# The seam between neighbouring pairs of an RWKV-style recurrence: first right sides around the low scores, turned answers and first answers ahead of the diagonal and the u-r scores

## The chip, the cores and the metric

The kernel runs on one core of one Trainium2 chip. The metric is the device time of one execution in microseconds (us). The core has TensorE (PE, with its weight loads PEld), VectorE (DVE), ScalarE (ACT), GpSimd (POOL) and SyncE (SP, which issues all the DMAs here). Each works through its own list in order, and they wait for each other by semaphores.

## What is computed

```python
def _attn_ref(r, k, v, w, a, b):           # 4 x 8 heads, 768 steps, head size 40
    for t in range(S):
        y[:, :, t] = np.einsum('bhd,bhde->bhe', rt, state)
        Sa = np.einsum('bhde,bhe->bhd', state, at)
        state_decay = state * wt[:, :, None, :] - np.einsum('bhd,bhe->bhde', Sa, bt)
        state = state_decay + np.einsum('bhd,bhe->bhde', vt, kt)
    return y
# x: y as (3072 tokens, 320)
# first MLP:  h = x @ w_in (2048);  x = (h - tanh(h)) @ w_out
# experts:    out = sum over 4 of  p_e * (relu(x @ w1[e]) @ w2[e]), inner size 1024
```

## The kernel before, in words

The sequence is cut into 6 chunks of 128 steps. A unit is one chunk of 4 heads; there are 48 units, worked in 24 pairs (pair `p` holds units `2p` and `2p+1`, called `j` = 0 and 1). Four pairs (`PPC`) make a chunk. Within a chunk the recurrence becomes a triangular system, solved in four blocks of 32 steps, b = 0 to 3. For each block and each `j` this chain runs:

- PE, `right_sides` (L569 with the state, L572 with the values) and, for b > 0, `right_side_rest` (L585, with the answers found so far and the low scores): the right side in a bank.
- DVE, `save_right_side` (L1052): right side to `rhs`.
- PE, `answer` (L595): `rhs` times the inverse of the diagonal block.
- ACT, `save_answer` (L868): answer to `un`.

Around that chain, per pair: `scores` (L708, L712) masked by DVE `mask_scores` (L1076); `scores_low` (L723), saved by ACT in three pieces (`save_low`, L885); `natural` (L736), saved by L892; `turn_state` (L610), saved by L874; `turn_answers` (L622), saved by ACT to `ut` (`save_turned_answers`, L879); `scores_ur` (L687, from `ut` and r), masked by DVE `mask_ur` (L1067); `state_by_values` (L634) and `state_by_answers` (L642), added by DVE `update_state` (L1061) and decayed by POOL (L1189); results (L658, L667, L675), saved by DVE (L1086).

`diagonal(i)` (L549) forms the diagonal blocks of a unit that was prepared some pairs ahead: DVE scan (L991) and reciprocal (L997), POOL scaling (L1178, L1181), diagonal on PE, `save_diagonal` on ACT (L863). Pairs 0 and 1 prepare three units each, pair 2 none, pairs 3 to 18 two each, later ones none; the diagonals follow one pair later.

The order on each engine is written out by hand. `program` calls, for p = 0 to 23, the engine's `pair(p)` and, at a chunk's end, its `mlp` for the chunk before. So pairs 7, 11, 15, 19 and 23 are followed by an MLP of 16 steps on PE (`drained(p)` is true for them), in which the u-r scores and results of that pair are finished (L814 up, L823 down). The other 19 seams p to p+1 join two pairs directly. On ACT a pair may end with more work: in pairs 3 to 6 `weight_hi`, the casts of two pieces of MLP weights (L900 to L902, which wait for DMAs), and in pairs 9, 13, 17 and 21 `tokens_hi`, the casts of turned tokens (L909, L910). After pair 3 DVE computes the rest of the inverses of the next chunk (L1027, L1030).

After the last MLP come the experts (L1383, L1393, ACT L1418, DVE L1448 and L1455), from about 830 us to the end.

At a direct seam PE's list before reads `scores_low(p+1)`, `turn_answers(p)`, both first right sides, a wait for `update_state`, one diagonal, `scores_ur(p)`, both first answers, both right sides of block 1, `turn_state`, the second diagonal, `right_side_rest` of block 1.

Of the kernel before, what the change touches and what calls it, by code (L numbers as in the profile page):

```python
# [142 lines left out]
def recurrence_and_first_mlp(nc, sem, pairs, ident, kbaw, rvt, vn, w_in, w_out, scratch, turned, middle):  # L143
    ctx = ExitStack()
    with ctx:
# [58 lines left out]
        def rows(s):  # L204
            return slice(HALF * s, HALF * s + HD)
# [5 lines left out]
        def block_of(b):  # L211
            return slice(BLK * b, BLK * (b + 1))
# [13 lines left out]
        def drained(p):  # L226

            return p % PPC == PPC - 1 and p >= PPC
# [306 lines left out]
        def _(pe):  # L535
            def diagonal(i):

                _, b_made, a_made, _ = parts(i)
                o = diagonal_of(i)
                pe.wait_ge(scaled, 2 * (i + 1))  # L540
                if i in late_diagonals:
                    pe.wait_ge(ut_saved, (i - FIRST) // 2 + 1)
                elif i >= FIRST:
                    pe.wait_ge(lt_saved, i)
                elif i >= 2:
                    pe.wait_ge(lt_saved, i - 1)
                for b in range(NB):
                    for h, q, s in heads:
                        mm = pe.matmul(o[block_of(h), block_of(b)], b_made[rows(s), 1, q, block_of(b)],  # L549
                                       a_made[rows(s), q, block_of(b)], start=True, stop=True)  # L550
                mm.then_inc(lt_full, 1)
# [198 lines left out]
            def pair(p):  # L750
                after_mlp = p > 0 and drained(p - 1)
                prepared = [] if after_mlp else prepared_in(p - 1)
                more = p + 1 < NP
                right_sides(p, 0, 0)
                right_sides(p, 1, 0)
                if after_mlp:
                    pe.wait_ge(x2_saved_v, 2 * (p // PPC - 1))
                    pe.wait_ge(x2_saved_a, 2 * (p // PPC - 1))
                if p:
                    pe.wait_ge(st_read, p)  # L760
                for i in prepared[:1]:
                    diagonal(i)
                if p and not after_mlp:
                    scores_ur(p - 1)
                answer(p, 0, 0)
                answer(p, 1, 0)
                right_sides(p, 0, 1)
                right_sides(p, 1, 1)
                turn_state(p)
                for i in prepared[1:2]:  # L770
                    diagonal(i)
                right_side_rest(p, 0, 1)
                right_side_rest(p, 1, 1)
                for i in prepared[2:]:
                    diagonal(i)
                state_by_values(p)
                answer(p, 0, 1)
                answer(p, 1, 1)
                if p and not after_mlp:
                    result_by_answers(p - 1)  # L780
                right_sides(p, 0, 2)
                right_sides(p, 1, 2)
                right_side_rest(p, 0, 2)
                right_side_rest(p, 1, 2)
                if more:
                    scores(p + 1, 0)
                answer(p, 0, 2)
                answer(p, 1, 2)
                result_by_keys(p)
                right_sides(p, 0, 3)  # L790
                right_sides(p, 1, 3)
                right_side_rest(p, 0, 3)
                right_side_rest(p, 1, 3)
                result_by_state(p)
                answer(p, 0, 3)
                answer(p, 1, 3)
                if more:
                    natural(p + 1, 0)
                    scores(p + 1, 1)
                state_by_answers(p)  # L800
                if more:
                    natural(p + 1, 1)
                    scores_low(p + 1)
                turn_answers(p)

            passes = [(HI0, HI0), (HI0, LO0), (LO0, HI0), (HI1, HI1), (HI1, LO1), (LO1, HI1), (ST2, ST2), (ST2, LO2)]

# [49 lines left out]
        def _(act):  # L857
# [62 lines left out]

            def pair(p):
                prepared = [] if p and drained(p - 1) else prepared_in(p - 1)
                for i in prepared[:1]:
                    save_diagonal(i)
                save_answer(p, 0, 0)
                save_answer(p, 1, 0)
                save_turned_state(p)
                for i in prepared[1:]:
                    save_diagonal(i)
                for b in range(1, NB):  # L930
                    save_answer(p, 0, b)
                    save_answer(p, 1, b)
                if p + 1 < NP:
                    save_natural(p + 1, 0)
                    save_natural(p + 1, 1)
                if p + 1 < NP:
                    save_low(p + 1)
                save_turned_answers(p)
                if 0 <= p - PIECES_FROM < PIECES // 2:
                    weight_hi(2 * (p - PIECES_FROM))  # L940
                    weight_hi(2 * (p - PIECES_FROM) + 1)
                if tokens_turned_in(p) is not None:
                    tokens_hi(tokens_turned_in(p))
# [555 lines left out]
```

## Time and profile before

| | |
|---|---|
| three timed runs | 1687.89 us median (1684.33, 1687.89, 1695.4) |
| the profiled execution | 1691.96 us, its span 1690.3 us |
| PE busy | 1485.6 us (88%) |
| PEld busy | 1295.8 us (77%) |
| DVE busy | 810.7 us (48%) |
| ACT busy | 421.0 us (25%) |
| POOL busy | 375.2 us (22%) |
| mean granted TensorE clock | 0.946 |

The span is the time from the first to the last instruction. Matmuls are pipelined, so a busy PE is not one at its peak. In the timeline a row is a run of like instructions: its start, how long it lasts, engine, line, operands, how many (matmuls of 32-bit numbers are shown as two), and in square brackets how long the engine had been idle before it and what released it. "Granted clock" is the share of 2.4 GHz that TensorE was allowed; it has two levels, 2.4 and 1.2 GHz.

### The profile page before, as it was taken

Reading aid. Unit: us, or ns where it says so; the run is one execution under the profiler, and the core shown is the slowest. Engines: PE = TensorE matmul, PEld = TensorE weight load, DVE = VectorE, ACT = ScalarE, POOL = GpSimd, SP = SyncE. Lnnn points to the kernel's source line nnn. Section 1 sums busy time; section 2 is a strip of 40 time slices with the busy share of each in tenths; the row PEclk is TensorE's granted clock in tenths of the full one; section 3 lists DMA queues with packets and bytes.
Section 4 is the critical chain, followed back from the end, with each engine's and each line's share of the span. In section 5 each row is a group of like instructions: output and inputs, shape, how many; then the busy total and the mean of one; then the engine's idle time right before and its main releaser. Section 6 shows DMA issues by size and latency. Waiting matters only on the chain. (4 is left out here: it accounts for less than half of the span.)

```text
span 1690.3 us, 37880 instructions
## 1 busy us (share of the span) xinstructions
PE 1485.6 (88%) x15888; PEld 1295.8 (77%) x15888; DVE 810.7 (48%) x1395; ACT 421.0 (25%) x859; POOL 375.2 (22%) x314
## 2 busy tenths in 40 slices
PE   1288466998998998999997789999999999999998
PEld 0166355876877886887786669999999999999998
DVE  6876844866866776663211243333333333333333
ACT  0033233333333334323322231111111111111111
POOL 4131254333333323231132440202020202010000
PEclk9987677999999998997898989999999999999999
DMA  6544466136226316212000140100000010100011
GB/s 184 142 127 120 112 197 171 34 100 183 62 73 186 86 54 155 65 35 60 9 8 27 48 147 19 26 8 20 14 11 23 1 33 0 34 0 0 0 47 47
DMA packets 89411, 112.84 MB, mean 67 GB/s; under 512 B 10952, under 2 KB 67400, under 8 KB 89288
## 3 DMA queue, kind: packets, MB, share of 16 engines
q1 hardware_dynamic: 89288, 111.05, 23.4%
q8 instruction: 96, 1.57, 0.4%
q14 instruction: 27, 0.22, 0.0%
HBM read 78.73 MB, written 32.28 MB: 66 GB/s over the span
## 5 line engine op out<-in xcount | busy, mean ns | idle before, releaser
L1383 PE MATMUL banks<-x2t,u 128*128 x1536 | 377.9, 393 | 8.2 <-POOL u L1350 8.2
L1393 PE MATMUL banks<-u,hid 128*128 128x320 f32 x2304 | 360.6, 309 | 0.0
L1393 PEld LDWEIGHTS banks<-u,hid 128*128 128x128 f32 x2304 | 349.0, 188 | 11.2
L1448 DVE SCALAR_TENSOR_TENSOR hid<-banks,hid 128x512 fp32r<-128x512 f32 x192 | 132.9, 692 | 414.1 <-ACT hid L1418 414.1
L1383 PEld LDWEIGHTS banks<-x2t,u 128*128 128x128 f32 x1536 | 284.4, 189 | 61.3 <-issue 8.5
L1418 ACT ACTIVATE hid<-banks 128x512 fp32r<-128x512 f32 x192 | 115.0, 599 | 581.5 <-PE banks L1383 581.5
L814 PE MATMUL banks<-xt,wi 128*128 128x512 f32 x768 | 198.3, 401 | 19.9 <-issue 12.8
L823 PE MATMUL banks<-wo,hid 128*128 128x320 f32 x1152 | 183.8, 309 | 5.7 <-POOL hid L1220 5.7
L823 PEld LDWEIGHTS banks<-wo,hid 128*128 128x128 f32 x1152 | 175.4, 188 | 14.2 <-POOL hid L1220 6.4
L814 PEld LDWEIGHTS banks<-xt,wi 128*128 128x128 f32 x768 | 142.8, 192 | 48.1 <-issue 21.2
L1220 POOL TENSOR_TENSOR hid<-gap,hid 128x512 fp32r<-128x512 f32 x96 | 123.8, 1289 | 227.4 <-ACT hid L957 227.1
L1146 DVE TENSOR_TENSOR gap<-banks,gap 128x512 f32<-128x512 f32 x96 | 66.1, 689 | 140.6 <-ACT gap L950 140.4
L1455 DVE SCALAR_TENSOR_TENSOR acc<-banks,pn,acc 128x320 f32 x192 | 92.5, 546 | 60.3 <-PE banks L1393 60.3
L950 ACT ACTIVATE gap<-banks 128x512 f32<-128x512 f32 x96 | 57.6, 600 | 239.3 <-PE banks L814 237.9
L1052 DVE TENSOR_TENSOR rhs<-banks,own 128x160 f32<-128x160 f32 x192 | 53.3, 318 | 131.0 <-PE banks L585 126.3
L1178 POOL TENSOR_TENSOR made<-made 104x512 f32<-104x512 f32 x42 | 53.6, 1276 | 274.2 <-DVE made L997 274.2
L1342 POOL CAST u<-raw 128x1024 fp32r<-128x1024 f32 x8 | 8.3, 1042 | 476.2 <-PE banks L1393 455.6
L868 ACT ACTIVATE un<-banks 32x160 f32<-32x160 f32 x192 | 56.8, 296 | 214.5 <-PE banks L595 212.0
L595 PE MATMUL banks<-rhs,tt 128*32 128x160 f32 x384 | 55.4, 357 | 53.8 <-DVE rhs L1052 53.4
L1027 DVE TENSOR_TENSOR ld<-ld,tmp 128x31 f32<-128x31 f32 (+15 forms) x186 | 88.2, 474 | 5.3
L1076 DVE TENSOR_TENSOR nvmak<-banks,upper 128x1024 f32<-128x1024 f32 x48 | 58.6, 1220 | 38.4 <-PE banks L712 38.4
L1030 DVE TENSOR_TENSOR tmp<-tt,ld 128x31 f32<-128x31 f32 (+15 forms) x155 | 73.0, 471 | 4.5
(105 smaller groups left out, 1552.5 us busy)
## 6 DMA issues: line engine op xcount, KB each, us to landing
scaled_operands<-made SPq DMA_DIRECT2D x42, 416.8 KB
made<-kbaw SPq DMA_DIRECT2D x42, 312.0 KB
kb<-scaled_operands SPq DMA_DIRECT2D x24, 416.0 KB
raw<-w SPq DMA_DIRECT2D x8, 640.0 KB, 5.5
lam<-scaled_operands SPq DMA_DIRECT2D x24, 209.6 KB
at<-scaled_operands SPq DMA_DIRECT2D x24, 208.0 KB
raw<-w SPq DMA_DIRECT2D x8, 512.0 KB, 4.0
rt<-rvt SPq DMA_DIRECT2D x96, 40.0 KB
```

Source lines behind the costliest of these rows:

```text
L814: mm = pe.matmul(solve_bank(f % 2), wi[:, w, part], xt[:, x, :], start=(n == 0), stop=(n == 7))
L823: mm = pe.matmul(down_bank[t][:, 0:D], hid[:, f % HIDS, h, part], wo[:, w, f, :], start=(f == 0 and n == 0), stop=(f == NF1 - 1 and n == 2))
L1027: ins = dve.tensor_tensor(out=ti[:, j + 1:, 0:ncol], in0=ti[:, j + 1:, 0:ncol], in1=t, op=ALU.subtract)
L1030: ins = dve.tensor_tensor(out=t, in0=bc(lu[:, j + 1:, j:j + 1], [128, nr, ncol]), in1=bc(ti[:, j:j + 1, 0:ncol], [128, nr, ncol]), op=ALU. ...
L1076: dve.tensor_tensor(out=nvmak[:, j, :, :, :, :].rearrange("p s a q t -> p s (a q) t"), in0=score_pair[:, :, :].rearrange("p s (k t) -> p s ...
L1146: dve.tensor_tensor(out=gap[:, f % 2, :], in0=solve_bank(f % 2), in1=gap[:, f % 2, :], op=ALU.subtract)\
L1220: pool.tensor_tensor(out=hid[:, f % HIDS, 1, :], in0=gap[:, f % 2, :], in1=hid[:, f % HIDS, 0, :].bitcast(F32), op=ALU.subtract).then_inc( ...
L1383: mm = pe.matmul(p_up[f][:], u1[:, par, w, f * 128:(f + 1) * 128], xt[:, x, cols], start=(i == 0), stop=(i == 7))
L1393: mm = pe.matmul(p_dn[t][:, 0:D], hid[:, f, h, t * 128:(t + 1) * 128], u2[:, par, w, f, :], start=(f == 0 and i == 0), stop=(f == NFU - 1 ...
L1418: act.activation(hid[:, f, 0, :], p_up[f][:], ACT.Relu).then_inc(e_hi, 1)
L1448: dve.scalar_tensor_tensor(out=hid[:, f, 1, :], in0=p_up[f][:], scalar=0.0, in1=hid[:, f, 0, :].bitcast(F32), op0=ALU.max, op1=ALU.subtract)\
L1455: dve.scalar_tensor_tensor(out=a, in0=p_dn[t][:, 0:D], scalar=pn[:, bass.ds(n * BATCH + t, 1), bass.ds(e, 1)] .rearrange("p o e -> p (o e) ...
```

## The change

At a direct seam (not after an MLP), on PE:

- the first right sides of unit j = 0 of the next pair go ahead of `scores_low(p+1)`, those of j = 1 behind it;
- `turn_answers(p)` follows them (it is now called at the head of the next pair);
- the two first answers come next, then the wait for `update_state`, the diagonal, the right sides of block 1, and only then `scores_ur(p)`, followed by `turn_state`.

On ACT `save_turned_answers(p)` moves from the end of the block of scores in pair p to the head of pair p+1, and the two first `save_answer` go ahead of `save_diagonal`. DVE, POOL and SP keep their lists. No instruction is added or removed.

```diff
@@ PE, pair(p)
-                right_sides(p, 0, 0)
-                right_sides(p, 1, 0)
+                if p == 0 or after_mlp:
+                    right_sides(p, 0, 0)
+                    right_sides(p, 1, 0)
+                else:
+                    turn_answers(p - 1)
                 if after_mlp:
                     pe.wait_ge(x2_saved_v, 2 * (p // PPC - 1))
                     pe.wait_ge(x2_saved_a, 2 * (p // PPC - 1))
+                answer(p, 0, 0)
+                answer(p, 1, 0)
                 if p:
                     pe.wait_ge(st_read, p)
                 for i in prepared[:1]:
                     diagonal(i)
+                right_sides(p, 0, 1)
+                right_sides(p, 1, 1)
                 if p and not after_mlp:
                     scores_ur(p - 1)
-                answer(p, 0, 0)
-                answer(p, 1, 0)
-                right_sides(p, 0, 1)
-                right_sides(p, 1, 1)
                 turn_state(p)
...
                     natural(p + 1, 1)
+                    if not drained(p):
+                        right_sides(p + 1, 0, 0)
                     scores_low(p + 1)
-                turn_answers(p)
+                    if not drained(p):
+                        right_sides(p + 1, 1, 0)
+                if drained(p):
+                    turn_answers(p)
@@ ACT, pair(p)
+                if p and not drained(p - 1):
+                    save_turned_answers(p - 1)
+                save_answer(p, 0, 0)
+                save_answer(p, 1, 0)
                 for i in prepared[:1]:
                     save_diagonal(i)
-                save_answer(p, 0, 0)
-                save_answer(p, 1, 0)
                 save_turned_state(p)
...
                     save_low(p + 1)
-                save_turned_answers(p)
+                if drained(p):
+                    save_turned_answers(p)
                 if 0 <= p - PIECES_FROM < PIECES // 2:
                     weight_hi(2 * (p - PIECES_FROM))
```

PE at the seam from pair 8 to pair 9, before, from the low scores (L723) to the first answers (L595); L569 and L572 here are the first right sides of j = 0 and 1, L549 the diagonal, L687 the u-r scores:

```order
L723 MATMUL banks<-at,kb 96x96 x8
L622 MATMUL banks<-ident,un 104x128 x4
L569 MATMUL banks<-st,at 32x40 x4
L572 MATMUL banks<-vnat,nvmak 32x40 x4
L569 MATMUL banks<-st,at 32x40 x4
L572 MATMUL banks<-vnat,nvmak 32x40 x4
L549 MATMUL banks<-made 32x32 x16
L687 MATMUL banks<-rt,ut 128x128 x8
L595 MATMUL banks<-rhs,tt 32x160 x2
```

The same place in the changed kernel, from the low scores to the turned state (L610); the last four L569 and L572 are the right sides of block 1:

```order
L723 MATMUL banks<-at,kb 96x96 x8
L569 MATMUL banks<-st,at 32x40 x4
L572 MATMUL banks<-vnat,nvmak 32x40 x4
L622 MATMUL banks<-ident,un 104x128 x4
L595 MATMUL banks<-rhs,tt 32x160 x2
L549 MATMUL banks<-made 32x32 x16
L569 MATMUL banks<-st,at 32x40 x4
L572 MATMUL banks<-vnat,nvmak 32x40 x4
L569 MATMUL banks<-st,at 32x40 x4
L572 MATMUL banks<-vnat,nvmak 32x40 x4
L687 MATMUL banks<-rt,ut 128x128 x8
L610 MATMUL banks<-ident,st 104x104 x4
```

The answers L595 moved from behind the diagonal and the u-r scores to ahead of both, and the u-r scores L687 stand directly ahead of the turned state.

ACT before, where pair 4 ends with two pieces of weights (L900 to L902) and pair 5 begins:

```order
L885 ACTIVATE low<-banks 32x8x32
L879 ACTIVATE ut<-banks 104x512
L900 ACTIVATE wi<-spare 128x2x256
L901 ACTIVATE wi<-spare 128x256
L902 ACTIVATE wo<-spare 128x640
L900 ACTIVATE wi<-spare 128x2x256
L901 ACTIVATE wi<-spare 128x256
L902 ACTIVATE wo<-spare 128x640
L863 ACTIVATE ld<-banks 128x128
L868 ACTIVATE un<-banks 32x4x40 x2
```

The same place in the changed kernel, whose line numbers on ACT are 8 higher (L893 is the low scores' copy, L908 to L910 the weights, L887 `ut`, L876 the answers, L871 the diagonal):

```order
L893 ACTIVATE low<-banks 32x8x32
L908 ACTIVATE wi<-spare 128x2x256
L909 ACTIVATE wi<-spare 128x256
L910 ACTIVATE wo<-spare 128x640
L908 ACTIVATE wi<-spare 128x2x256
L909 ACTIVATE wi<-spare 128x256
L910 ACTIVATE wo<-spare 128x640
L887 ACTIVATE ut<-banks 104x512
L876 ACTIVATE un<-banks 32x4x40 x2
L871 ACTIVATE ld<-banks 128x128
```

The copy to `ut` moved from ahead of both pieces of weights to behind them. At the ends of pairs 9, 13, 17 and 21 it moves behind L909 and L910 in the same way.

## Rows read from the trace of the kernel before

**Rows 1.** Busy time by stretch: us, each engine's busy (instructions), PEclk granted clock, DMA

```profile
100.00:145.00 45.00, 36.84 (x778) 29.23 (x780) 28.13 (x47) 11.01 (x31) 10.47 (x12) 0.70 0.47 126
192.00:300.00 108.00, 79.91 (x1630) 63.52 (x1632) 49.82 (x84) 38.45 (x91) 43.70 (x40) 0.79 0.59 165
352.00:427.00 75.00, 66.17 (x1599) 53.81 (x1600) 48.55 (x80) 28.81 (x73) 23.18 (x23) 0.98 0.62 165
```

**Rows 2.** Timeline of PE, seam of pairs 8 and 9

```profile
368.95 0.92 PE L723 MATMUL banks<-at,kb 40*96 40x96 f32 x16 [0.23 <-DVE nvmak L1076]
369.81 0.64 PE L622 MATMUL banks<-ident,un 128*104 128x128 f32 x4
...
371.12 0.46 PE L549 MATMUL banks<-made 40*32 40x32 f32 x32 [0.24 <-DVE st L1061]
372.38 1.16 PE L687 MATMUL banks<-rt,ut 40*128 40x128 f32 x16 [0.81 <-ACT ut L879]
373.48 0.35 PE L595 MATMUL banks<-rhs,tt 128*32 128x160 f32 x2
...
374.21 0.57 PE L610 MATMUL banks<-ident,st 104*104 104x104 f32 x4
...
375.57 0.66 PE L634 MATMUL banks<-vnat,kbn 128*64 128x40 f32 x16
...
385.86 0.92 PE L723 MATMUL banks<-at,kb 40*96 40x96 f32 x16 [0.23 <-DVE nvmak L1076]
```

**Rows 3.** Timeline of DVE, seams of pairs 0 and 1 and of 8 and 9

```profile
102.91 0.56 DVE L1052 TENSOR_TENSOR rhs<-banks,own 128x160 f32<-128x160 f32 x2
...
370.48 0.59 DVE L1061 TENSOR_TENSOR st<-banks,st 40x160 f32<-40x160 f32 x2
371.10 0.56 DVE L1052 TENSOR_TENSOR rhs<-banks,own 128x160 f32<-128x160 f32 x2
...
373.59 1.23 DVE L1067 TENSOR_TENSOR nu<-banks,upper 128x1024 f32<-128x1024 f32 x1 [0.65 <-PE banks L687]
375.44 0.56 DVE L1052 TENSOR_TENSOR rhs<-banks,own 128x160 f32<-128x160 f32 x2 [0.62 <-PE banks L585]
```

**Rows 4.** Timeline of ACT, last weight cast of pair 4, then seams 8-9 and 9-10

```profile
217.36 0.72 ACT L902 ACTIVATE wo<-spare 128x640 fp32r<-128x640 f32 x1
...
371.74 0.60 ACT L879 ACTIVATE ut<-banks 104x512 f32<-104x512 f32 x1
...
389.14 1.05 ACT L909 ACTIVATE xt<-spare 128x1024 fp32r<-128x1024 f32 x1
390.08 0.62 ACT L910 ACTIVATE xt<-spare 128x512 fp32r<-128x512 f32 x1
```

**Rows 5.** Timeline of PE, seams with a long wait: pairs 0-1, 3-4, 4-5

```profile
103.29 0.71 PE L595 MATMUL banks<-rhs,tt 128*32 128x160 f32 x2 [1.59 <-DVE rhs L1052]
...
104.73 0.94 PE L610 MATMUL banks<-ident,st 104*104 104x104 f32 x4
...
192.61 0.62 PE L595 MATMUL banks<-rhs,tt 128*32 128x160 f32 x2 [19.35 <-DVE rhs L1052]
...
213.34 0.56 PE L610 MATMUL banks<-ident,st 104*104 104x104 f32 x4
218.38 0.65 PE L549 MATMUL banks<-made 40*32 40x32 f32 x32 [4.48 <-ACT ld L863]
```

**Rows 6.** Timeline of PE, seams without diagonals: pairs 20-21 and 22-23

```profile
769.13 1.16 PE L687 MATMUL banks<-rt,ut 40*128 40x128 f32 x16 [1.55 <-ACT ut L879]
...
808.65 2.08 PE L687 MATMUL banks<-rt,ut 40*128 40x128 f32 x16 [1.55 <-ACT ut L879]
...
811.88 0.94 PE L610 MATMUL banks<-ident,st 104*104 104x104 f32 x4
```

**Rows 7.** Timeline of PE, low scores at seams 16-17 and 17-18

```profile
632.74 0.92 PE L723 MATMUL banks<-at,kb 40*96 40x96 f32 x16 [0.23 <-DVE nvmak L1076]
...
652.17 0.92 PE L723 MATMUL banks<-at,kb 40*96 40x96 f32 x16 [0.23 <-DVE nvmak L1076]
```

## The prediction

> **What bounds the kernel now.** I read the busy time by stretch first, then the timeline of PE at each kind of seam, then DVE and ACT at the same instants. The last chain of waits lies wholly in the experts, which the change leaves alone, so what is won or lost among the pairs moves the end one for one. PE is the engine that is nearly full: 66.17 of 75 us in the stretch of pairs 8 to 11 at a granted clock of 0.98, but 36.84 of 45 and 79.91 of 108 us in the early stretches at 0.70 and 0.79 [rows 1]. In a steady pair (16.91 us from low scores to low scores) PE's idle time lies at the seam, in three pieces: 0.23 us for the score mask, 0.24 us for the state, 0.81 us for `ut` [rows 2]. That is 1.28 us, the most a steady seam can give.
>
> Some seams are different. At 0-1 PE waits 1.59 us for the first right sides, since DVE prepares a third unit first; at 3-4 it waits 19.35 us for the inverse on DVE; at 4-5 it waits 4.48 us behind the weight casts on ACT [rows 5]. At 20-21 and 22-23 no diagonal is left and the wait for `ut` is 1.55 us [rows 6].
>
> **The change, seam by seam.** All durations are steps from one row's start to the next.
>
> *Steady seams* (8-9, 10-11, 12-13, 14-15, 16-17, 18-19: six). Low scores start at 368.95 as before, because they wait for the mask; j = 0's right sides fill the gap ahead. Low scores take 0.86, j = 1's right sides about 0.17, the turned answers 0.57: PE is free at 370.55. The first answers need DVE's `rhs`, started at 371.10, right behind the state update at 370.48 [rows 2, 3]. DVE's list has not changed, so that stays. From DVE's start to the answer is 0.38 us (102.91 to 103.29 [rows 3, 5]), so the answers start at 371.48, after about 0.9 us of idle. Then: answers and block 1's right sides 0.8 (0.73 in 373.48 to 374.21, a little more because j = 1's `rhs` comes later), diagonal 0.4, u-r scores 1.10, which makes turned state at about 373.8 against 374.21. `ut` is saved at 372.34 [rows 4], just before it is wanted at 372.7, so that wait is gone: it moved to `rhs`. DVE's mask of u-r scores was 1.21 behind their start and lasts 1.23, so it would end at 375.1 and let block 1's `rhs` start at 375.15 against 375.44 [rows 3]. Gain 0.3 to 0.4, I take 0.35: six times, **-2.1 us**.
>
> *Token seams* (9-10, 13-14, 17-18, 21-22). ACT's casts L909 and L910, 0.94 and 0.53 from start to start, now lie ahead of the copy to `ut` [rows 4]. `ut` is 1.47 us later, and queued behind it are u-r scores and turned state on PE and their mask on DVE, for which block 1 waits. Ahead of that wait PE now does the answers and right sides, 0.73. Net 0.74 each; at 21-22, where that work takes 1.2 at the lower clock (from 808.65 to 811.88 less about 2.0 of u-r scores [rows 6]), 0.25. **+2.4 us**.
>
> *Seams 20-21 and 22-23*: `ut` is as early as before, answers and right sides now precede it, so turned state comes 0.73 to 1.2 us earlier. **-1.95 us** for the two.
>
> *Seam 2-3*: DVE, which runs parts of an inverse between its saves there, sets the pace of that pair. I take **0** (below nothing: at most -0.6, the steady gain with the later `ut`).
>
> *Seams 0-1 and 1-2.* Before, diagonal and u-r scores ran while PE waited for `rhs`. Now they stand behind the answers that wait for it, so they are exposed: 1.10 + 0.39 = 1.5 us at full clock. But PE comes out of that wait at the lower clock: turned state takes 0.94 at 104.73 against 0.57 [rows 5, 2], and u-r scores 2.08 against 1.16 [rows 6], which makes 2.6 us. A slow stretch that ends at the same time in both kernels returns the difference. Two seams, 3.0 to 5.2; middle, **+4.1 us**.
>
> *Seam 3-4*: the same two pieces behind 19.35 us of wait, 1.5 to 2.6; **+2.0 us**.
>
> *Weight seams 4-5, 5-6, 6-7.* This is the largest term. The copy to `ut` now stands behind two pieces of weights, the last of which starts at 217.36 and takes 0.72 [rows 4]. Before, PE had done u-r scores and turned state by 213.9 and waited at the second diagonal until 218.38 [rows 5]. Now it stops ahead of the u-r scores; `ut` is saved at 218.6, 0.24 us behind the old restart, and then u-r scores (1.10 or 2.0) and turned state (0.49 or 0.87) follow, in the open. Per seam 1.84 at full clock, 3.1 at half (the diagonal takes 0.65 there against 0.46 [rows 5, 2]); I take 2.5. Three seams: 5.5 to 9.3, **+7.5 us**. SP waits for the u-r scores before it loads r and a later unit, so these loads start some 3 us later, but what they feed is read a pair or more later. The weight loads follow loads of v that wait for scores late in the pair, so they shift with the pair and don't absorb its delay.
>
> The sum is 4.1 + 2.0 + 7.5 - 2.1 + 2.4 - 1.95 = **+12.0 us**; ends 7.6 and 16.2, taking each kind of seam at its own ends. The profiled execution took 1691.96 us, which gives 1704.0; it is 4.1 above the median of 1687.89. Over the four executions the mean is 1689.9, and I forecast from that: **1702 us**.
>
> The choice between full and half clock rests on when slow stretches end. From rows the exposed work costs between the two. The Trainium skill (TensorE: Matmul & The Clock Gate, HAM oscillation) speaks against putting work behind a wait: a PE that idles long between bursts restarts each burst throttled, and it advises to finish matmuls before waiting. By that page alone the three groups of long waits would take the slow price, 5.2 + 2.6 + 9.3, and the sum would be 15.5 instead of 12.0.
>
> **The rivals.**
>
> *The clock falls at more seams.* The short waits merge into one of 0.9 us at steady seams, and into 0.9 and about 1.1 at token seams. The pair after the low scores at 632.74 took 19.43 us instead of 16.91 [rows 7, 2], although that seam's waits were the usual ones, so the clock falls easily: 2.5 us each time. If it falls at six more of the nine steady and token seams with diagonals, that adds 15: +27, 1717 us. Against it: total idle at steady seams is smaller.
>
> *The clock falls less, and the kernel is not slower.* The seams whose wait for `ut` was 1.55 us (rows show 20-21 and 22-23) came with slow stretches, turned state 0.94 at 811.88 [rows 6]; 2-3 and 21-22 have the same wait. The change shortens it to about 1.2. If these four and the one at 632.74 are spared at 2.5 us each, -12.5 makes the sum -0.5: 1689 us. It decides from five spared stretches on. Against it: token seams, which get longer waits, are among them.
>
> *The weight seams hide their cost.* If pairs 4 to 6 are paced by landing weights, work exposed behind one wait is taken off the next: -7.5, 1694 us. For it: ACT's casts there wait for DMAs. Against: the loads are issued late in a pair, after its scores.
>
> **How the numbers follow.** Forecast (+7.6 to +16.2, so 1697 to 1706): 0.58. More clock falls: 0.22. Fewer: 0.12. Hidden weight seams: 0.08. The range 1689 to 1716 takes in the other cases but their far ends. A change of about 1%, 17 us, is what a measurement of this kernel can tell from none. Slower by more: nearly all of the first rival and the top of the forecast, 0.28. Faster by more: only a clock that rises well beyond its rival, 0.04. Within: 0.68.
>
> **What would show it.** After, PE should wait at a steady seam once, about 0.9 us, at L595 for `rhs`, with no wait for `ut`; the pair's pitch should be near 16.55. At 9-10 there should be a second wait of about 1.1 us at L687 and a pitch near 17.65. At 4-5 the wait should stand at L687 (6 to 7 us, released by ACT's `ut`), with turned state about 8 us later than before relative to low scores. At 0-1 the wait of some 4 us should stand at L595. I am wrong if the early stretches (to 300 us) don't grow by about 13.6, or if the later ones move by more than a few us either way, which would be the clock.

## The result and the profile after

The changed kernel took 1697.27 us (median of 22 runs, 1690.23 to 1706.2), the kernel before 1687.6 us (22 runs, 1679.56 to 1696.26). The ratio is 1.0058, with a 95% interval of 1.0041 to 1.0075: 9.8 us slower by the ratio, 9.7 by the medians. A later series of the same kernel gave 1.0056 (1.0037 to 1.0076). The forecast was 1702 us, and slower by less than 1%. The profiled executions took 1691.96 us before and 1697.88 after: the first lies 4.4 us above its median, the second 0.6, so these two profiles show some 4 us less of a difference than the runs.

| | before | after |
|---|---|---|
| span of the profiled execution | 1690.3 us | 1696.2 us |
| PE busy | 1485.6 us | 1483.9 us |
| DVE busy | 810.7 us | 809.7 us |
| ACT busy | 421.0 us | 421.5 us |
| mean granted TensorE clock | 0.946 | 0.949 |

The engines do the same work, so the time lies in waits. In the changed file the lines of the pairs on PE keep their numbers; those of ACT are 8 higher (`ut` L887, `un` L876, the weight casts L908 to L910, the token casts L917 and L918), those of DVE 11 higher (`rhs` L1063, `nu` L1078). The chain that ended last still lies in the experts.

Busy time by stretch of the changed kernel (us, each engine's busy time with its instructions, the granted clock, DMA share, GB/s):

```profile
100.00:145.00 45.00, 33.04 (x705) 25.89 (x704) 26.00 (x40) 11.50 (x30) 11.66 (x12) 0.66 0.45 119
192.00:300.00 108.00, 74.78 (x1632) 59.43 (x1632) 52.54 (x94) 36.08 (x86) 38.92 (x37) 0.74 0.58 162
...
755.00:820.00 65.00, 57.71 (x1176) 47.62 (x1174) 25.24 (x53) 24.26 (x56) 11.32 (x9) 0.97 0.22 62
```

Against [rows 1] PE does less in the first two stretches: 33.04 of 45 us for 36.84, 74.78 of 108 us for 79.91, at a lower clock. That is where the time goes. The last stretch holds pairs 20 to 22, of which more below; before, its clock was 0.77 to 0.79.

**A steady seam.** PE of the changed kernel, seam of pairs 8 and 9:

```profile
382.21 0.92 PE L723 MATMUL banks<-at,kb 40*96 40x96 f32 x16
...
384.73 0.72 PE L595 MATMUL banks<-rhs,tt 128*32 128x160 f32 x4 [0.75 <-DVE rhs L1063]
385.38 0.46 PE L549 MATMUL banks<-made 40*32 40x32 f32 x32
385.77 0.28 PE L569 MATMUL banks<-st,at 104*32 104x40 f32 x8
...
386.20 1.16 PE L687 MATMUL banks<-rt,ut 40*128 40x128 f32 x16
387.29 0.57 PE L610 MATMUL banks<-ident,st 104*104 104x104 f32 x4
```

The three waits of [rows 2] have become one of 0.75 us for `rhs`. None for `ut` is left. The turned state comes 5.08 us behind the low scores, where it was 5.26 (368.95 to 374.21 in [rows 2]). DVE of the changed kernel at that seam:

```profile
384.35 0.56 DVE L1063 TENSOR_TENSOR rhs<-banks,own 128x160 f32<-128x160 f32 x2
...
387.41 1.22 DVE L1078 TENSOR_TENSOR nu<-banks,upper 128x1024 f32<-128x1024 f32 x1 [1.20 <-PE banks L687]
388.55 0.54 DVE L1063 TENSOR_TENSOR rhs<-banks,own 128x160 f32<-128x160 f32 x2
```

Block 1's `rhs` starts as soon as DVE has masked the u-r scores, so the start of the u-r scores (386.20) now sets the pair. Before, block 1's `rhs` waited for PE's L585 instead, which stands behind the turned state [rows 3]. The u-r scores start later than they did, 3.99 us behind the low scores for 3.43, and still block 1's `rhs` comes a little earlier, at 6.34 us for 6.49. From low scores to low scores the pair takes 16.78 us (382.21 to 398.99), where it took 16.91.

**A token seam.** ACT, then PE, of the changed kernel at the seam of pairs 9 and 10:

```profile
401.77 1.06 ACT L917 ACTIVATE xt<-spare 128x1024 fp32r<-128x1024 f32 x1
402.74 0.61 ACT L918 ACTIVATE xt<-spare 128x512 fp32r<-128x512 f32 x1
403.38 0.60 ACT L887 ACTIVATE ut<-banks 104x512 f32<-104x512 f32 x1
```

```profile
398.99 0.92 PE L723 MATMUL banks<-at,kb 40*96 40x96 f32 x16
401.52 0.71 PE L595 MATMUL banks<-rhs,tt 128*32 128x160 f32 x4 [0.74 <-DVE rhs L1063]
...
404.02 2.00 PE L687 MATMUL banks<-rt,ut 40*128 40x128 f32 x16 [0.97 <-ACT ut L887]
405.95 0.93 PE L610 MATMUL banks<-ident,st 104*104 104x104 f32 x4
```

The copy to `ut` stands behind both casts, PE waits for it a second time (0.97 us), and here the u-r scores run at the lower clock (2.00 us for 1.16: 1.2 instead of 2.4 GHz). The next low scores start at 419.52: 20.53 us for a pair that took 16.92.

**A weight seam.** ACT, then PE, of the changed kernel at the seam of pairs 4 and 5:

```profile
224.50 0.63 ACT L908 ACTIVATE wi<-spare 128x512 fp32r<-128x512 f32 x1 [1.76 <-DMA spare<-w_out]
...
226.08 0.60 ACT L887 ACTIVATE ut<-banks 104x512 f32<-104x512 f32 x1
```

```profile
217.49 0.71 PE L595 MATMUL banks<-rhs,tt 128*32 128x160 f32 x4 [0.75 <-DVE rhs L1063]
...
226.73 2.08 PE L687 MATMUL banks<-rt,ut 40*128 40x128 f32 x16 [7.71 <-ACT ut L887]
228.74 0.93 PE L610 MATMUL banks<-ident,st 104*104 104x104 f32 x4
```

ACT still waits for the DMA of a piece of weights, but now the copy to `ut` waits with it. PE stands for 7.71 us ahead of the u-r scores, where it stood for 4.48 us behind them at the diagonal [rows 5]. Those scores and the turned state then run in the open at the lower clock: 2.01 and 0.86 us from start to start.

**A seam with a long wait, and one without diagonals.** PE of the changed kernel, seams of pairs 0-1, 3-4, 20-21 and 21-22:

```profile
104.71 0.98 PE L595 MATMUL banks<-rhs,tt 128*32 128x160 f32 x4 [4.40 <-DVE rhs L1063]
...
106.89 2.08 PE L687 MATMUL banks<-rt,ut 40*128 40x128 f32 x16
...
197.52 0.89 PE L595 MATMUL banks<-rhs,tt 128*32 128x160 f32 x4 [25.23 <-DVE rhs L1063]
...
784.39 1.16 PE L687 MATMUL banks<-rt,ut 40*128 40x128 f32 x16 [0.91 <-ACT ut L887]
785.48 0.57 PE L610 MATMUL banks<-ident,st 104*104 104x104 f32 x4
...
802.07 1.16 PE L687 MATMUL banks<-rt,ut 40*128 40x128 f32 x16 [2.52 <-ACT ut L887]
```

At 0-1 the whole wait stands ahead of the answers, and the u-r scores follow at half the clock. At 20-21 the wait for `ut` fell from 1.55 us [rows 6] to 0.91 us and the turned state took 0.57 us, at full clock. At 21-22, where `ut` stands behind the token casts, the wait is 2.52 us.

**Seam by seam.** The pitch is the time from one pair's low scores to the next pair's (by ACT's copies of them). Each part of the change was also run alone. Ten profiles (of the two kernels, the four parts, the changed kernel run again, `ut` first, the short waits only and the last three seams) give every seam in the old and in the new order; the table has their means. "New, `ut` first" is the new order with the copy to `ut` left ahead of ACT's casts.

| seam | old | new | new, `ut` first | predicted difference |
|---|---|---|---|---|
| 0-1 | 23.06 | 25.68 | | +2.05 (1.5 to 2.6) |
| 1-2 | 27.68 | 28.56 (27.96 without one at 30.36) | | +2.05 (1.5 to 2.6) |
| 2-3 | 18.11 | 18.38 (18.07 without one at 19.60) | | 0 |
| 3-4 | 42.58 | 45.77 | | +2.0 |
| 4-5 | 24.15 | 27.38 | 24.58 | +2.5 |
| 5-6 | 25.78 | 28.22 | 27.65 | +2.5 |
| 6-7 | 23.93 | 27.38 | 24.07 | +2.5 |
| 8-9, 12-13 | 16.91 | 16.75 | | -0.35 |
| 10-11 | 20.62 | 16.91 | | -0.35 |
| 14-15 | 19.95 | 17.69 | | -0.35 |
| 16-17 | 18.48 | 17.37 | | -0.35 |
| 18-19 | 17.76 | 16.75 | | -0.35 |
| 9-10 | 16.98 | 18.70 | 18.34 | +0.74 |
| 13-14 | 17.40 | 19.03 | 17.55 | +0.74 |
| 17-18 | 20.17 | 18.63 | 18.82 | +0.74 |
| 20-21 | 18.78 (16.46 at full clock) | 16.08 | | -0.73 to -1.2 |
| 21-22 | 19.51 (16.46 at full clock) | 19.04 | 16.08 | +0.25 |
| 22-23, to the MLP's first copy | 19.85 | 16.37 | | -0.73 to -1.2 |

One value rests on one to six profiles, and seams that now and then fall to the lower clock scatter by 2 to 4 us. No low scores follow pair 23, so its time runs from its own low scores to ACT's first copy of the MLP, `gap`. Added up, the columns differ by +6.7 us at the long waits, +9.1 at the weight seams, +1.3 at the token seams, -8.4 at the steady ones, -2.7 at 20-21, -3.5 at 22-23 and +0.3 at 2-3: about +3, beside 9.8 measured over many runs. The low scores of pair 1, ahead of all these seams, also start 2.0 us later in the four profiles with the new order at 0-1 (99.7 us for 97.7 on average), which no row explains. So the table shows which parts cost and which gain, but it doesn't add up to the whole.

### The profile page after: what moved, and what is told of

The parts are those of the page before. It is cut to its first block and busy times, and to the rows that moved or that the text cites. A ratio compares the mean times of both kernels' runs of the same rounds, so it can differ in the third digit from the quotient of the medians.

```text
span 1696.2 us, 37888 instructions
## 1 busy us (share of the span) xinstructions
PE 1483.9 (87%) x15888; PEld 1293.0 (76%) x15888; DVE 809.7 (48%) x1395; ACT 421.5 (25%) x859; POOL 375.1 (22%) x314
## 5 line engine op out<-in xcount | busy, mean ns | idle before, releaser
L595 PE MATMUL banks<-rhs,tt 128*32 128x160 f32 x384 | 57.4, 349 | 76.2 <-DVE rhs L1063 76.2
L876 ACT ACTIVATE un<-banks 32x160 f32<-32x160 f32 x192 | 56.4, 294 | 205.3 <-PE banks L595 203.0
L1063 DVE TENSOR_TENSOR rhs<-banks,own 128x160 f32<-128x160 f32 x192 | 53.4, 317 | 89.4 <-PE banks L585 87.4
L595 PEld LDWEIGHTS banks<-rhs,tt 128*32 128x32 f32 x384 | 24.2, 143 | 91.2 <-DVE tt L1047 50.3
```

Source lines behind the costliest of these rows:

```text
L595: pe.matmul(answer_bank[answer_rows(j, b), 0:GH * HD], tt[:, :, NB * g + b], rhs[:, j, :, :].rearrange("p h d -> p (h d)"), start=True, st ...
```

## Experiments

The kernels below carry one table, `NEW`: the seams p to p+1 that take the new order. `NEW = ()` is the order of the kernel before. Their lines for the same work are 2 higher on PE, 9 or 10 higher on ACT and 13 or 14 higher on DVE than in the changed kernel.

### Only the seams with a long wait

```diff
+NEW = (0, 1, 3)
```

> The new order at seams 0-1, 1-2 and 3-4 alone, the old one elsewhere. Theory A (work that stood ahead of a wait now stands behind it): turned state behind the wait for the first right sides comes 1.5 to 2.6 us later at each, +4 to +7 us in all (the two profiles gave pitches +3.3, +0.4 and +1.9). Theory B (the gain and loss of the whole change is mostly how often the clock falls): the waits here already restarted PE at the lower level before, so nothing changes, within 1.5 us of before.

Measured: 1691.88 us against 1683.62, ratio 1.0049 (1.0015 to 1.0083). That is 8 us, a little above the 4 to 7 of theory A: the seams alone do cost. But 1-2 did not cost what it was priced at. PE of this kernel at that seam (low scores, first answers, u-r scores, turned state, answers of blocks 1 and 2):

```profile
125.48 0.92 PE L725 MATMUL banks<-at,kb 40*96 40x96 f32 x16
131.66 0.97 PE L597 MATMUL banks<-rhs,tt 128*32 128x160 f32 x4 [4.40 <-DVE rhs L1077]
133.84 2.08 PE L689 MATMUL banks<-rt,ut 40*128 40x128 f32 x16
135.85 0.93 PE L612 MATMUL banks<-ident,st 104*104 104x104 f32 x4
142.23 0.97 PE L597 MATMUL banks<-rhs,tt 128*32 128x160 f32 x4 [2.26 <-DVE rhs L1077]
146.98 0.49 PE L597 MATMUL banks<-rhs,tt 128*32 128x160 f32 x4
```

The same place in the kernel before, whose low scores start at 119.77:

```profile
127.40 0.94 PE L610 MATMUL banks<-ident,st 104*104 104x104 f32 x4
133.79 0.97 PE L595 MATMUL banks<-rhs,tt 128*32 128x160 f32 x4 [2.26 <-DVE rhs L1052]
139.56 0.75 PE L595 MATMUL banks<-rhs,tt 128*32 128x160 f32 x4
```

From the low scores, the turned state is 10.37 us away, before it was 7.63: 2.7 us later, the slow price. Block 1's answers are 2.7 us later too. Block 2's are at +21.50 against +19.79, and they take 0.49 us where they took 0.75: PE is back at full clock a block earlier in its work. The clock rises 20.1 us behind the low scores, where it rose 22.9 us behind them before. That returns the cost; the pair is only 0.3 us longer (27.96 for 27.68) in three of four profiles. At 0-1 nothing of the kind happens, and the 2.6 us stay.

### Only the weight seams

```diff
+NEW = (4, 5, 6)
```

> The new order at seams 4-5, 5-6 and 6-7 alone. Theory A (copy to ut queued behind the weight casts on ACT, u-r scores and turned state exposed behind it): +5.5 to +9 us (the two profiles gave +3.5, -1.0, +3.8). Theory B (clock): these pairs restart slow in both kernels, so the slow stretches take up the exposed work, under +3 us.

Measured: 1695.37 us against 1683.62, ratio 1.0075 (1.0043 to 1.0107), the largest of the parts, as forecast, and by the ratio 12.6 us, more than the 5.5 to 9 of theory A (the pitches of this profile give 8.2). The cost isn't hidden by landing weights.

### Only the token seams

```diff
+NEW = (9, 13, 17, 21)
```

> The new order at seams 9-10, 13-14, 17-18 and 21-22 alone. Theory A: u-r scores 1.47 us later, 0.73 us of work moved ahead: +0.5 to +0.8 us each, +2.4 us in all, beyond that nothing. Theory B: the second wait of about 1 us at these seams brings the clock down at some of them, 2.5 us each time, so +5 to +10 us.

Measured: 1691.51 us against 1683.62, ratio 1.003 (1.0009 to 1.0052), so about 5 us by the ratio (7.9 by the medians), at the lower end of theory B. The pitches of these seams scatter: 9-10 took 17.78 us in two profiles and 20.53 in the third, where the clock fell behind the 0.97 us wait. 17.78 is near the predicted 17.65.

### Only the seams without casts

```diff
+NEW = (2, 8, 10, 12, 14, 16, 18, 20, 22)
```

> The new order at the seams with nothing behind the low scores on ACT: 2-3, 8-9, 10-11, 12-13, 14-15, 16-17, 18-19, 20-21, 22-23. Theory A: 0.12 to 0.35 us gained at each of the six steady ones, 0.7 to 1.2 at 20-21 and 22-23, none at 2-3: -3 to -4 us. Theory B: the shorter wait for ut spares slow stretches, so -5 to -10 us.

Measured: 1679.08 us against 1683.62, ratio 0.997 (0.9946 to 0.9994). The new order helps where no cast stands ahead of `ut`. The size, 5 us, lies between the two theories, and the interval reaches into both. Of it, the order by itself gives 0.15 us at each of the six steady seams and 0.38 us at 20-21 (16.08 for 16.46, both at full clock). Most of the rest comes with the clock. Busy time by stretch, 755 to 820 us, of this kernel, and 762 to 822 us of the kernel before:

```profile
755.00:820.00 65.00, 60.04 (x1087) 49.32 (x1078) 23.81 (x46) 24.53 (x56) 11.53 (x10) 1.00 0.14 36
```

```profile
762.00:822.00 60.00, 54.26 (x1050) 43.07 (x1046) 20.69 (x42) 20.32 (x47) 6.25 (x5) 0.77 0.17 45
```

Another part is neither order nor clock. At 10-11, the steady seam that gained most, PE of the kernel before stands for 2.69 us within pair 11, and the profile finds nothing that it waits for ("issue"):

```profile
414.61 0.20 PE L572 MATMUL banks<-vnat,nvmak 128*32 128x40 f32 x1 [2.69 <-issue]
```

All five profiles with the old order at this seam have such a wait there (0.49 to 2.71 us, 2.0 on average), none of the five with the new order has one. What it is, and why it went, isn't shown. In four of those five the clock fell within 2 us of its end. So of the 3.7 us that 10-11 gained, about 2 are this wait.

### The whole change, but `ut` copied ahead of the casts

```diff
 # ACT, end of pair p
-                if drained(p):
-                    save_turned_answers(p)
+                save_turned_answers(p)
                 if 0 <= p - PIECES_FROM < PIECES // 2:
                     weight_hi(2 * (p - PIECES_FROM))
```

(and `turn_answers` and the rest on PE as in the change; the call at the head of ACT's next pair is gone.)

> The whole change on PE, but ACT copies to ut at the end of the pair, ahead of the weight and token casts, as before. Theory A (the place of that copy in ACT's list is what the weight and token seams cost): the losses of the weight seams (about 8 us) and token seams (about 3) go, those of 0-1, 1-2 and 3-4 stay, so -1 to +4 us against before; pitches after the weight seams are as before, 23.5 to 28, and PE waits there at the diagonal for ld again. Theory B (PE's own new order costs it there): still +8 to +12 us.

Measured: 1679.25 us against 1685.95, ratio 0.9965 (0.9943 to 0.9988). One call back in its old place on one engine turns 0.6% slower into 0.35% faster, more than theory A allowed (-1 to +4 us): in this profile the clock didn't fall once from pair 9 to the end of pair 23. PE of this kernel at the seam of pairs 4 and 5 (answers, u-r scores, turned state, second diagonal):

```profile
222.32 0.72 PE L597 MATMUL banks<-rhs,tt 128*32 128x160 f32 x4 [0.75 <-DVE rhs L1077]
...
223.78 1.16 PE L689 MATMUL banks<-rt,ut 40*128 40x128 f32 x16
224.88 0.56 PE L612 MATMUL banks<-ident,st 104*104 104x104 f32 x4
231.28 0.65 PE L551 MATMUL banks<-made 40*32 40x32 f32 x32 [5.84 <-ACT ld L881]
```

The wait for ACT is back behind the turned state, and nothing that it exposes is on the way to block 1 but the second diagonal, as before the change. The pitches of 4-5 and 6-7 are 24.58 and 24.07 us, near the old 24.15 and 23.93. 5-6 took 27.65 us in this one profile, near the new value; why isn't shown.

### The other side: the old order, `ut` late at the weight seams

```diff
 # ACT; PE keeps the order of the kernel before
+                if p - 1 in (4, 5, 6):
+                    save_turned_answers(p - 1)
...
-                save_turned_answers(p)
+                if p not in (4, 5, 6):
+                    save_turned_answers(p)
```

> PE's old order everywhere; only ACT's copy to ut moves behind the weight casts at seams 4-5, 5-6, 6-7. Theory A (the place of the copy on ACT is the cost): PE stops at the u-r scores, and these, the first answers, right sides and turned state follow in the open, +2.5 to +4.5 us a seam, +8 to +13 us. Theory B (PE's new order is the cost): within 3 us of before.

Measured: 1697.32 us against 1687.41, ratio 1.0075 (1.0046 to 1.0105). PE of this kernel at the seam of pairs 4 and 5:

```profile
222.27 2.08 PE L689 MATMUL banks<-rt,ut 40*128 40x128 f32 x16 [8.27 <-ACT ut L897]
```

This moves nothing on PE and costs as much as the weight seams of the change (1.0075 both). The pitches of 4-5, 5-6 and 6-7 are 28.04, 29.69 and 27.99 us, 3.9 to 4.1 above the old ones: behind the late `ut` the old order exposes the first answers too, so PE's new order softens this cost to some 3 us a seam. With the run before, this shows the cause of the largest term from both sides: it is the place of one copy in ACT's list, not PE's order.

### New order only where the wait is short, `ut` first

```diff
+NEW = (2, 8, 9, 10, 12, 13, 14, 16, 17, 18, 20, 21, 22)
```

> The new order with the copy to ut ahead of the casts, at all direct seams but 0-1, 1-2, 3-4 and the weight seams. Theory A: what is left is only gain, 0.15 us at steady seams, 0.15 to 0.7 at token seams, 1 to 3 at those without diagonals: -4 to -8 us. Theory B: no better than the run with the plain seams alone, -5 us or less.

Measured: 1672.12 us against 1685.95, ratio 0.9921 (0.9887 to 0.9955). Leaving the long waits and the weight seams in the old order gives about another 7 us over the kernel with `ut` first everywhere (13.8 for 6.7 against the same runs). That is well beyond the 4 to 8 us of theory A. The two intervals overlap, so the difference is likely rather than shown. The long seams' two additions (2.6 at 0-1, 3.2 at 3-4) are of that size.

### Weight casts behind the answers of the next pair

```diff
 # ACT, pair(p); PE keeps the order of the kernel before
                 for b in range(1, NB):
                     save_answer(p, 0, b)
                     save_answer(p, 1, b)
+                    if 0 <= p - 1 - PIECES_FROM < PIECES // 2 and b < 3:
+                        weight_hi(2 * (p - 1 - PIECES_FROM) + b - 1)
...
-                if 0 <= p - PIECES_FROM < PIECES // 2:
-                    weight_hi(2 * (p - PIECES_FROM))
-                    weight_hi(2 * (p - PIECES_FROM) + 1)
```

> The old order at every seam; only ACT's weight casts move, from the end of pairs 3 to 6 to behind the answers of blocks 1 and 2 in pairs 4 to 7. Theory A (the weight casts, which wait for DMAs at the head of ACT's list, are themselves the large cost at these seams, 4.5 to 7 us each of three): -10 to -16 us, the pitches after seams 4-5 to 6-7 fall from 23.5-28 to 17-20. Theory B (the casts only move, and the DMA wait then holds back the answers of blocks 2 and 3): -3 to +5 us.

Measured: 1696.6 us against 1685.95, ratio 1.0053 (1.0023 to 1.0082): slower by 9 us, and a miss for both expectations. The pairs from 4-5 on took 30.71, 21.05 and 31.87 us where they took 23.75, 28.21 and 23.64. DVE of this kernel in pair 5, then PE:

```profile
222.88 2.04 DVE L1015 TENSOR_TENSOR_SCAN made<-made 104x128 f32<-104x128 f32 x2 [11.58 <-DMA made<-kbaw]
```

```profile
225.19 0.98 PE L597 MATMUL banks<-rhs,tt 128*32 128x160 f32 x4 [7.38 <-DVE rhs L1076]
```

DVE waits 11.58 us for the load of a later unit (`kbaw`), whose scan stands ahead of the last `rhs` in DVE's list, and PE waits behind it. ACT's own wait didn't go either (4.82 us for a piece of `w_out` at 214.02). What had worked was seam 3-4: pair 4 took 36.8 us for 42.6, so that the low scores of pair 5 started at 200.85 instead of 208.08. But the load was issued no earlier than in the kernel before (215.22, where it was 215.03). The reason lies in the lists of POOL and SP, which the edit left alone. POOL, then SP, of this kernel:

```profile
193.20 1.27 POOL L1222 TENSOR_TENSOR wi<-spare,wi 128x512 fp32r<-128x512 f32 x1 [22.90 <-ACT wo L920]
...
201.02 1.27 POOL L1202 TENSOR_TENSOR made<-made 104x512 f32<-104x512 f32 x1
```

```profile
215.22 0.32 SPq L202 DMA_DIRECT2D made<-kbaw  x1
```

POOL's part of the weights waits for ACT's casts (22.90 us), and the scaling of the prepared unit (L1202) stands behind it. SP waits for that scaling before it stores the unit (202.96, where it was 200.06), and its later loads, of v, weights and `kbaw`, follow in order. So the moved casts held back POOL, SP and with them the load, while the pair had moved ahead. The run doesn't tell what late casts are worth with POOL's and SP's lists moved along.

### All that had looked good together

```diff
+NEW = (2, 4, 5, 6, 8, 9, 10, 12, 13, 14, 16, 17, 18, 20, 21, 22)
```

(with `ut` first, and the weight casts late as in the run before)

> The new order at all direct seams but 0-1, 1-2 and 3-4, with the copy to ut ahead of other casts, and the weight casts behind the answers of blocks 1 and 2 of the next pair. Theory A: the sum of the two previous ones, -14 to -24 us. Theory B: no better than the late weight casts alone.

Measured: 1677.16 us against 1685.95, ratio 0.9951 (0.9927 to 0.9975). That is 8 us faster, which neither theory named (-14 to -24, or no better than the run before). It doesn't beat the version with short waits only, and the late casts show no gain here either.

### Only the last three seams

```diff
+NEW = (20, 21, 22)
```

(`ut` first)

> The new order at seams 20-21, 21-22 and 22-23 alone, ut ahead of the token casts. Theory A (only the idle time itself moves, 0.7 to 1.2 us a seam): -2 to -3.5 us. Theory B (the shorter wait for ut also spares the slow stretches of the last chunk, whose pitches went from 19.1-20.6 to 16.1 in the earlier profiles): -7 to -11 us, granted clock about 1.00 in that chunk against 0.80.

Measured: 1681.25 us against 1687.41, ratio 0.997 (0.9944 to 0.9995), a size between those of the theories; the pitches tell more. Busy time by stretch, 755 to 820 us, and PE at the seam of pairs 20 and 21:

```profile
755.00:820.00 65.00, 60.84 (x1222) 49.21 (x1217) 26.54 (x52) 25.07 (x57) 9.94 (x9) 1.00 0.17 45
```

```profile
779.80 1.16 PE L689 MATMUL banks<-rt,ut 40*128 40x128 f32 x16 [0.91 <-ACT ut L897]
```

Two seams whose wait for `ut` went from 1.55 to 0.91 us now run at 16.08 us each, where the profiled execution before had 19.10 and 20.42. The granted clock of the stretch is 1.00; that of the kernel before, over 762 to 822 us, was 0.77. The order itself is worth 0.38 us a seam (16.46 at full clock in the old order). So most of what these seams pay goes with the clock. Over all fourteen profiles, the clock fell in the old order at 20-21 in three of six, at 21-22 in five of six and at 22-23 in six of six; where the wait for `ut` was 0.91 us it fell in none of eight, five and eight. The wait for the mask of the scores (0.23 us) went too, and no run takes the two apart.

### The diagonal ahead of the first answers

The version with short waits only, with one more move, on PE alone (ACT's list stays, with the answers ahead of the diagonal):

```diff
 # PE, head of a pair in the new order
-                answer(p, 0, 0)
-                answer(p, 1, 0)
                 if p:
                     pe.wait_ge(st_read, p)
                 for i in prepared[:1]:
                     diagonal(i)
+                answer(p, 0, 0)
+                answer(p, 1, 0)
                 right_sides(p, 0, 1)
```

> As the run with the short seams and ut first, but the diagonal ahead of the first answers. Theory A (at a steady seam PE is idle 0.75 us for rhs, and the diagonal, ready at the state update just before, fits in most of it): turned state 0.3 to 0.5 us earlier, pitch 16.3 to 16.5 instead of 16.75, -1 to -4 us beyond that run, so about -14 to -18 us against before. Theory B (block 1's right side waits for DVE's mask of the u-r scores, which ut sets): same pitch, 0 beyond it.

Measured: 1669.07 us against 1687.41, ratio 0.9897 (0.9861 to 0.9933). This is faster than both kernels, by 17 to 18 us against the one before. PE at the seam of pairs 8 and 9:

```profile
368.78 0.92 PE L725 MATMUL banks<-at,kb 40*96 40x96 f32 x16
...
370.95 0.46 PE L551 MATMUL banks<-made 40*32 40x32 f32 x32 [0.39 <-DVE st L1085]
371.33 0.55 PE L597 MATMUL banks<-rhs,tt 128*32 128x160 f32 x3
...
372.24 1.16 PE L689 MATMUL banks<-rt,ut 40*128 40x128 f32 x16
373.33 0.56 PE L612 MATMUL banks<-ident,st 104*104 104x104 f32 x4
...
385.03 0.92 PE L725 MATMUL banks<-at,kb 40*96 40x96 f32 x16
```

The diagonal waits for the state only, which is ready 0.6 us before `rhs`, so it fills the wait: 0.39 us is left of 0.75. The turned state comes 4.55 us behind the low scores, and the pair takes 16.25 us where the changed kernel has 16.75 and the old one 16.91. The steady seams 12-13, 16-17 and 18-19 show the same 0.5 us. By the totals alone this version isn't told from the one with short waits only (0.9921), whose interval overlaps.

### The changed kernel again

The changed kernel's order written with the table (`NEW` holds all 19 seams), as a common measure for the parts.

> The changed kernel again, instruction for instruction, beside the others. If the parts measured alone (+8.2, +12.6, +5.0, -5.0, together +20.8) add up, +18 us or more; if the separate totals carry a few us of chance in clock and fetch waits each, +8 to +13 us as first measured.

Measured: 1693.9 us against 1687.41, ratio 1.0056 (1.0037 to 1.0076), the same as the changed kernel. The four parts alone give 0.49 + 0.75 + 0.30 - 0.30 = 1.24%, the whole 0.56%. They were all measured against one set of runs of the kernel before, with a median of 1683.62, which was 1685.95 and 1687.41 in the two later sets; a common error of 0.15% would enter the sum four times and close the gap. That this is the reason isn't shown.

## Why the prediction was right, and where it was off

**The sign and size.** +12.0 us forecast, +9.8 measured (+9.4 by the repeat). The forecast held a change of 1% for what a measurement can tell from none; the interval shows that 0.6% is told. The early part came as forecast: the low scores of 8-9 start at 382.21 for 368.95, 13.3 us later, for "about 13.6". Of that, 1.4 us had arisen before the first changed seam (98.52 for 97.10), so the seams themselves made 11.8. The later part was predicted to move little without a change of clock. It gave back 7.3 us (the span is only 5.9 longer): 2.8 up to the low scores of pair 23 and 4.1 within pair 23, which ran at the lower clock for 10.2 us before and not at all after. Some 4 us of these 7.3 are the draw of the two profiles, as said above.

That the total came so near is in part luck. What the runs show without the gains of the clock is +6.7 and +9.1 at the early seams, about +2.4 at the token seams, -0.9 at the steady ones and -0.8 at 20-21 and 22-23: +16.5, by estimate. The clock and the "issue" waits, which the sum put at nothing, returned the rest, some 7 us by the measured 9.8.

**The weight seams, +7.5.** Right in place, cause and nearly size: the wait stood at L687, was released by ACT's `ut`, and the turned state was 13.8 us behind the low scores (214.96 to 228.74), which is 8.5 more than the 5.3 of a seam without that wait, for a predicted 8. The pitches say +9.1. The choice of 2.5 between 1.84 and 3.1 was too low: the u-r scores and the turned state ran at the lower clock at the traced seam (2.08 and 0.93 us), as the slow price assumed, and the slow price of 3.1 a seam was the better estimate (9.1 for 9.3). The Trainium skill (TensorE: Matmul & The Clock Gate, HAM oscillation) says that each burst behind a long idle restarts throttled. The trace agrees here: behind 7.71 us of wait the u-r scores took 2.08 us for 1.16. The rival that landing weights hide the cost is refuted by the two runs that touch these seams alone.

**The long waits, +6.1.** The sum was right (+6.7), its terms weren't. 0-1 paid 2.6, the slow price. For 1-2 the step that failed is the use of "A slow stretch that ends at the same time in both kernels returns the difference": I named it and then priced both seams alike. At 1-2 the slow stretch even ended earlier in the pair: 2.7 us late at the turned state, 0.3 at the pair's end. 3-4 paid 3.2 for 2.0; its wait, now ahead of all that work, grew from 19.35 to 25.23 us, but `rhs` came as far behind the low scores as before (27.0 us for 27.1). The extra goes with the moment at which the clock rose. It rose 35.2 us behind the low scores in the kernel before and 35.7 in the changed one, whose pitch is 44.44, 1.9 above the old; in two other profiles it rose at 38.8 (45.7) and in the fourth at 42.4 (47.26).

**The steady seams, -2.1.** The mechanism held: one wait of 0.75 us at L595, none for `ut`. The gain was 0.15 us each, not 0.35. The step "answers and block 1's right sides 0.8" failed: they take 0.65 and 0.43 from start to start, 1.08. In the old order these pieces had run into each other in 0.73 us. Block 1's `rhs` did come to wait for the mask of the u-r scores, as forecast, but these started 3.99 us behind the low scores, not 3.75, and `rhs` at 6.34, not 6.20. The pitches gained 8.4 us in all; the 7.5 beyond the order are the clock and, at 10-11, the "issue" wait.

**The token seams, +2.4.** The second wait of about 1.1 us came as 0.97. A seam at full clock took 17.78 (predicted 17.65). Some ran at the lower clock behind it (20.53 and 20.33), while the steady seams after them were faster. In the net, +1.3 by the pitches and 5 us by the run of these seams alone: the true size isn't settled.

**Seam 2-3, 0.** It held: 18.07 us for 18.11 in four of five profiles.

**20-21 and 22-23, -1.95.** The step "answers and right sides now precede it, so turned state comes 0.73 to 1.2 us earlier" was too large: 0.38 at full clock. The wait fell by 0.64 us, and these seams gained from the clock instead: 2.7 us at 20-21 and 3.5 at 22-23, order and clock together.

**The clock.** Of the rivals, "the clock falls less" is what happened in part. At 10-11, 14-15, 16-17, 18-19 and 20-21 the old order averaged 17.8 to 20.6 us, the new one 16.1 to 17.7. With 22-23 the pitches gained 14.6 us where the sum had 4.05 for these seams. That is 10.6 us more, near the 12.5 of that rival. The kernel stayed slower all the same, since the early seams took 15.8 us for 13.6, and since the measured total is some 7 us above what the pitches add up to. By the pitches the clock and the "issue" wait gave some 13 us beyond the order's 1.7, by the total some 7; which holds for the mean run isn't settled. The forecast had it as a rival with a chance of 0.12 and as a whole case; it should have stood in the sum as a term.

## What to carry to other kernels

When an instruction moves on an engine that works in order, look first at what it now stands behind: a copy that others wait for, put behind a cast that waits for a DMA, cost 0.75% by itself; with the same copy behind the token casts it was the whole difference between a slower and a faster kernel. Ready work belongs ahead of the wait, not behind it: the best order here was the one that put the diagonal, ready 0.6 us before `rhs`, into the gap, and the long waits were probably better left with their cover (7 us, with intervals that overlap). When a cast moves on one engine, look at what the others have queued behind it: here POOL's scaling and SP's loads were held back. And compare pitches seam by seam over several profiles: a total of +0.6% was made of parts of +9 and -8 us, and even the pitches of ten profiles didn't add up to it.

## What the runs showed of the hardware

The granted clock reacts to small changes of the waits. At 20-21 one wait of 1.55 us before the u-r scores (with the others of the seam) went with pairs of 19.1 to 20.4 us in three of six profiles, in the kernel before with a clock of 0.77 over the stretch; one of 0.91 us left the pair at 16.1 us in all eight. At 9-10 the waits were 0.74 and 0.97 us, and the clock fell in one of three; at the three token seams with diagonals together it fell in four of nine.

A stretch at the lower clock doesn't always cost what it stretches: 2.4 of the 2.7 us lost at the head of pair 2 were back at its end, since the answers of block 2 already took 0.49 us instead of 0.75.

PE can stand for 2.7 us where the profile finds nothing that it waits for. At 10-11 this took 0.49 to 2.71 us in each of five profiles with the old order and nothing in the five with the new one.
